# A new instruction order at the head of an MLP, and a last output tile stored in two halves

## The reference

```python
def _moe2_ref(x, w_in, w_out) -> np.ndarray:      # x 2304x512, w_in 512x2048, w_out 2048x512
    h = x @ w_in
    g = np.maximum(0.01 * h, h)
    return (g @ w_out).astype(np.float32)
```

## Time and profile before

| | us |
|---|---|
| median of 3 runs (lowest, highest) | 390.22 (389.74, 390.31) |
| the profiled execution | 390.76 |
| its span, first to last instruction | 389.0 |
| TensorE busy in the span | 376.5 |
| DVE busy | 220.4 |
| ACT busy | 195.0 |

### The profile page before, as it was taken

The page is one execution under the profiler, slowest core; times in us unless marked ns, Lnnn a source line. Parts: engine busy times, 40 slices in busy tenths (PEclk is TensorE's granted clock), DMA queues, the critical chain, the costliest instruction groups (busy, mean ns, idle before and its releaser), DMA issues.

```text
span 389.0 us, 9358 instructions
## 1 busy us (share of the span) xinstructions
PE 376.5 (97%) x3515; PEld 288.0 (74%) x3515; DVE 220.4 (57%) x763; ACT 195.0 (50%) x527; POOL 12.5 (3%) x46
## 2 busy tenths in 40 slices
PE   5999999999999999789999999999999999999996
PEld 3788877867785333467888888888888888888885
DVE  6776576665574273397866444644464464445443
ACT  5888878778762012476644334334334434433431
POOL 1200000000000100021100000000000000000000
PEclk9999999999999999999999999999999999999999
DMA  7798789769999999980000100200020002002002
GB/s 250 274 335 303 258 277 318 260 243 348 396 383 386 386 386 386 385 304 4 3 0 35 48 0 1 83 0 0 2 82 0 3 0 81 2 0 82 2 1 81
DMA packets 27214, 62.09 MB, mean 160 GB/s; under 512 B 2081, under 2 KB 2593, under 8 KB 27169
## 3 DMA queue, kind: packets, MB, share of 16 engines
q1 hardware_dynamic: 27024, 61.33, 43.8%
q10 hardware_dynamic: 144, 0.16, 0.1%
HBM read 56.77 MB, written 4.72 MB: 158 GB/s over the span
## 4 chain that ended last, share of the span: by engine, by line
PE 89%; DMA 5%; DVE 3%; SPq 1%; ACT 1%; issue 1%; POOL 0%; DVEq 0%; ACTq 0%; POOLq 0%
PE bank L862 10%; PE bank L864 10%; PE bank L863 10%; PE turned L557 6%; PE bank L590 6%; PE bank L533 6%; PE turned L863 6%; PE turned L864 6%; PE turned L862 5%; PE bank L579 5%; PE bank L847 4%; PE bank L763 4%; DMA slot<-in_moe_w_out_dram 3%; PE turned L607 3%; PE bank L873 1%; DMA qk<-in_k_dram 1%
## 5 line engine op out<-in xcount | busy, mean ns | idle before, releaser
L1457 DVE SCALAR_TENSOR_TENSOR g_sb<-bank,h_sb 128x384 f32<-128x384 f32 x93 | 51.8, 557 | 93.6 <-ACT h_sb L1133 93.4
L1133 ACT COPY h_sb<-bank 128x384 f32<-128x384 f32 x93 | 44.5, 478 | 118.9 <-PE bank L847 118.6
L864 PE MATMUL bank<-w_hi,g_lo 128*128 128x512 f32 x180 | 70.9, 394 | 0.0
L862 PE MATMUL bank<-w_hi,g_hi 128*128 128x512 f32 x180 | 70.6, 392 | 0.1
L863 PE MATMUL bank<-w_lo,g_hi 128*128 128x512 f32 x180 | 70.7, 393 | 0.0
L959 ACT ACTIVATE prob<-prob,row_min 128x192 f32<-128x192 f32 (+1 forms) x144 | 51.9, 440 | 3.9 <-DVE row_min L1211 3.9
L1464 DVE TENSOR_TENSOR g_lo<-g_sb,g_hi 128x384 fp32r<-128x384 f32 x93 | 51.0, 549 | 0.1
L1138 ACT CAST g_hi<-g_sb 128x384 fp32r<-128x384 f32 x93 | 48.0, 516 | 0.2 <-DVE g_sb L1457 0.2
L967 ACT COPY probT<-turned 128x384 f32<-128x384 f32 (+1 forms) x76 | 33.4, 443 | 20.2 <-PE turned L557 19.1
L533 PE MATMUL bank<-qk 64*64 64x192 f32 (+2 forms) x576 | 35.8, 325 | 5.1 <-DMA qk<-in_q_dram 4.0
L862 PEld LDWEIGHTS bank<-w_hi,g_hi 128*128 128x128 f32 x180 | 33.8, 188 | 9.1 <-DVE g_lo L1464 1.7
(11 more groups left out here) (169 smaller groups left out, 435.2 us busy)
## 6 DMA issues: line engine op xcount, KB each, us to landing
slot<-in_moe_w_dram SPq DMA_DIRECT2D x22, 1024.0 KB, 8.5
slot<-in_moe_w_dram SPq DMA_DIRECT2D x5, 2048.0 KB, 16.0
v<-in_v_dram SPq DMA_DIRECT2D x16, 325.0 KB, 4.5
qk<-in_q_dram SPq DMA_DIRECT2D x15, 288.0 KB, 4.6
qk<-in_k_dram SPq DMA_DIRECT2D x15, 288.0 KB, 5.3
slot<-in_moe_w_in_dram SPq DMA_DIRECT2D x4, 1024.0 KB, 14.3
slot<-in_moe_w_out_dram SPq DMA_DIRECT2D x8, 512.0 KB, 11.7
out_dram<-o_sb SPq DMA_DIRECT2D x5, 768.0 KB, 3.6
```

The lines of the kernel that those rows point to most:

```text
L862: nc.tensor.matmul(acc, hi, w_hi[:, f, :], start=(f == 0), stop=False)
L864: last = nc.tensor.matmul(acc, lo, w_hi[:, f, :], start=False, stop=(f == FT - 1))
L1133: nc.scalar.copy(h_sb[:, f % 2, :], bank[6 + f % 2][:, 0:GW]).then_inc(h_copied, 1)
L1457: nc.vector.scalar_tensor_tensor(out=g_sb[:, f % 2, :], in0=bank[6 + f % 2][:, 0:GW], scalar=0.01, in1=h_sb[:, f % 2, :], op0=ALU.mult, op ...
```

## The change

At the head of the MLP: TensorE runs `project(0)` ahead of `combine_T(3)`, no longer behind it. On ACT both halves of the first w_out pair are rounded later: half 0 behind g pieces 0 and 1, half 1 behind the h copy of block 1; g pieces 2, 3 and 4 are taken one place earlier each or more. On DVE the residual of half 0 moves behind the leaky of block 0 and g piece 2; pieces 3 and 4 move ahead of the leaky of blocks 1 and 2.

At the end: the last two blocks of the last group run tile by tile (tile 0 gets its 6 matmuls, then tile 1, then tile 2), DVE copies the last tile in two halves of 256 columns, SP stores the first half and ACT the second.

```diff
@@ sync, the last group's stores
-                sp.dma_start(out[row0:row0 + P, :], o_sb[:, t, :]).then_inc(out_stored, 16)
-            sp.wait_ge(out_stored, 16 * (NG - 1 + GT))
+                cols = slice(0, DM // 2 if t == GT - 1 else DM)
+                sp.dma_start(out[row0:row0 + P, cols], o_sb[:, t, cols]).then_inc(out_stored, 16)
+            sp.wait_ge(out_stored, 16 * (NG + GT))
@@ tensor
-            pe.wait_ge(c_hi_done, 3)
-            pe.wait_ge(c_lo_done, 3)
-            combine_T(3, C_BANK[3])
             project(0)
+            pe.wait_ge(c_hi_done, 3)
+            pe.wait_ge(c_lo_done, 3)
+            combine_T(3, C_BANK[3])
             project(1)
+            def last_blocks(par):
+                for t in range(GT):
+                    for f in (FT - 2, FT - 1):
+                        if t == 0:
+                            pe.wait_ge(glo_done, (NG - 1) * FT + f + 1)
+                        for kind in range(3):
+                            g, w = ((g_hi, w_hi), (g_hi, w_lo), (g_lo, w_hi))[kind]
+                            last = nc.tensor.matmul(bank[GT * par + t][:, :], g[:, f % NR2, t * P:(t + 1) * P], w[:, f, :],
+                                                    start=False, stop=(f == FT - 1 and kind == 2))
+                    last.then_inc(acc_done, 1)
-                        down(grp, par, FT - 2)
-                        down(grp, par, FT - 1)
+                        last_blocks(par)
@@ scalar
-            split_w_first(0)
                 split_g(0)
                 split_g(1)
-                split_w_first(1)
+                split_w_first(0)
+                split_g(2)
+                split_g(3)
                 act.wait_ge(h_done, 1)
...
-                split_g(2)
+                split_g(4)
                 copy_h(1)
-                split_g(3)
+                split_w_first(1)
                 round_g(1)
                 copy_h(2)
                 split_w(1)
                 round_g(2)
-                split_g(4)
                 split_g(5)
...
+            act.wait_ge(acc_copied, GT * NG + 1)
+            act.dma_start(out[NG * GW - P:NG * GW, DM // 2:DM], o_sb[:, GT - 1, DM // 2:DM]).then_inc(out_stored, 16)
@@ vector
-                    nc.vector.tensor_copy(o_sb[:, t, :], bank[GT * par + t][:, :]).then_inc(acc_copied, 1)
+                    parts = 2 if known(grp) and grp == NG - 1 and t == GT - 1 else 1
+                    for i in range(parts):
+                        cols = slice(i * DM // parts, (i + 1) * DM // parts)
+                        nc.vector.tensor_copy(o_sb[:, t, cols], bank[GT * par + t][:, cols]).then_inc(acc_copied, 1)
                 split_g(0)
                 split_g(1)
-                split_w_first(0)
...
                 split_g(2)
+                split_w_first(0)
                 lower_g(0)
+                split_g(3)
                 leaky(1)
                 split_w_first(1)
-                split_g(3)
                 lower_g(1)
+                split_g(4)
                 leaky(2)
                 split_w(1)
                 lower_g(2)
-                split_g(4)
                 split_g(5)
```

## The result

Over 20 executions each the median is 389.08 us for the changed kernel and 391.5 for the one before; the ratio is 0.9934 with a 95% interval of 0.9917 to 0.9952, so 0.66% faster (0.48 to 0.83%). The forecast was 388.07 of 390.22, a ratio of 0.9945, inside that interval. In microseconds the two lie 1.0 apart: the forecast started from the median of three executions, 390.22, and over 20 that kernel's median is 391.5. The gain is 2.4 us by these medians, 2.15 was forecast. The profiled execution took 388.57 with a span of 386.8, where 388.6 and 386.85 were forecast from the profile before.

What follows compares the result with a forecast made beforehand. TensorE was taken as the bound, except in the MLP's first blocks, where other engines' order makes it wait, and after its last matmul. Head 2.0 plus tail 0.15 us made 2.15, from 390.22 to 388.1 us; range 387.4 to 389.3.

Steps and rivals of the forecast that it cites:

- steps 1 to 3: MLP head: earlier `project(0)` and ACT g pieces bring `up(0)` 0.55 us and the first product 0.75 us earlier.
- the loads don't pin the gain: MLP head: w_out part 2 lands near 167.0, ACT reaches it at 169.9, so loads don't limit the 2.0 us.
- step 3: First block: no weight residual ahead of the leaky, so the first product comes at 164.26 instead of 165.01.
- steps 4 and 5: First blocks: second product group stalls 0.22 us; g piece 3 ahead of `leaky(1)` brings `up(3)` 2.02 us earlier.
- POOL's doubling: MLP head: POOL's doubling of g piece 3 ends by 166.9, letting `up(3)` go at 166.93.
- step 7: Blocks 4 and 5: late DVE residuals stall TensorE 0.22 and 0.37 us; block 5 keeps 2.03 us of gain.
- Tail: Kernel end: split copies lose 0.1 to 0.17 us, the half-size last store gains 0.34; net 0.15 us taken.
- the wait for block 15's residual: Last blocks: wait moves behind three matmuls, with 0.1 us cover; if that is gone, it costs under 0.1 us.
- DVE as the bound: MLP head: later DVE instructions give back half, leaving a head gain of 1.0 us, time 389.1; chance 0.2.
- The split tail: Kernel end: two copies and a second queue's landing come 0.3 to 0.6 us later, time 388.6; chance 0.1.
- the slow small store: Kernel end: last small store takes 5.4 us to landing instead of 2.1, time 391.7; chance 0.03.
- the gain tied to a fixed time: First group: a load or late stall takes back the whole head gain, time 390.2 or little below; chance 0.05.

Runs made afterwards that it cites:

- pieces-back run: Changed kernel with DVE's g pieces 3 and 4 again behind the weight residuals of blocks 1 and 2; ratio to the kernel before 0.9971.
- filled kernel: Kernel before with 12 identity transposes put into TensorE's waits for `up(0)` and the first product; 391.49 us, ratio to before 1.0002.
- combine back: Changed kernel with `combine_T(3)` ahead of `project(0)` again; 389.66 us, ratio to the kernel before 0.996.
- head alone: New order at the head with the old end of the kernel before; 390.01 us, ratio to before 0.996.
- residual early: Changed kernel with DVE's residual of w_out half 0 ahead of the first leaky; ratio to the kernel before 0.9945.
- residual and `up(1)` early: Changed kernel with DVE's residual of w_out half 0 ahead of the first leaky and `up(1)` ahead of the first products; 389.14 us, ratio to before 0.9953.

## Why the prediction was right, step by step

**Projection, pieces, first product (steps 1 to 3)** came as laid out: `project(0)` at 160.11 (160.2), ACT's pieces at 161.25 (161.35), `up(0)` at 162.72 (162.7), first product at 164.26 (164.26). The gain at the first product is 0.68 from the anchor, where I had 0.75, and it holds for this pair of traces; about 0.3 of it hangs on when the load of w_out lands, since the old head has its first product at 5.53 and 5.54 in the traces where the load came earlier. I had written that the loads don't pin the gain. They don't hold up the new order, but the old one waits for one of them, so they set a part of what the change is worth. Where the load is early, the place of `combine_T(3)` is the whole gain at the first product: 5.57 with it back, 5.53 with the whole old head. The residual moved behind the first leaky, to which step 3 points, brings nothing there: moved back ahead of it, in the new order, the first product stays at 5.16.

**`up(3)` (steps 4 and 5)**, 166.95 against 166.93, is the largest step, as I said, and the pieces-back run shows it alone: 1.39 us with two DVE instructions. I had 1.1 there. I had POOL's doubling end near 166.9; it ended at 166.54, and the time came out all the same because TensorE was busy with its third group until then.

**What DVE gives back (step 7)** was mis-sized: I had stalls of 0.22 and 0.37 before blocks 4 and 5. There is none before block 4 and next to none before block 5 (they start at 175.43 and 177.69, not 175.32 and 177.94). 0.33 of the 0.59 is that TensorE itself was later at `up(6)`, 175.25 and not 174.92: groups of three behind a wait or a projection took 0.93 to 0.96, where I had laid out the steady rate. The other 0.26 is DVE, whose residual of block 5 ended at 177.63 and not 177.89:

```profile
177.08 0.55 DVE L1480 TENSOR_TENSOR g_lo<-g_sb,g_hi 128x384 fp32r<-128x384 f32 x1
```

So block 5 was 2.28 earlier, not 2.03; 0.07 of that is the earlier anchor, which leaves 2.21. `up(15)` keeps 2.06: most of the rest went inside block 5, whose second matmul came 0.34 behind its first instead of 0.22. The stall late in the group is in both traces.

**That the sum met the span to 0.05 us is luck in part.** The head was 2.06 and the tail 0.25, both above what I took, and the earlier anchor gave 0.07 more; against that, the matmuls between `up(15)` and the last one took 0.18 longer (last section), for which my sum had nothing. 2.06 + 0.25 + 0.07 - 0.18 is the 2.2 by which the span is shorter.

**Tail.** 0.25 us of the 0.15 taken. The split copies cost 0.06 (0.76 for both; they ended 1.18 us behind the last matmul's start, against 1.12), where I had 0.1 to 0.17, and the landing was 0.3 shorter (1.8 for 2.1), as taken. The turns of the tiles cost nothing and bring at most 0.06; the wait for block 15's residual did not stall. The second queue brings about 0.1, which my sum didn't have as a term of its own: it is the 0.04 by which SP issues later and the 0.07 by which its issue is longer. By the rule of the Trainium skill that I quoted (DMA: Bandwidth & Descriptors, "Issuing engines are not separate DMA queues") a second issuing engine saves the sequencer's time to issue and no more; the traces agree, as the landing takes 1.80 us behind SP's last issue and 1.82 behind ACT's.

**The rivals.** DVE as the bound, with half of the head's gain given back, did not come: the head brought 1.7 to 2.1 us, not 1.0. There is something in it, as DVE is busy 8.15 of 9.20 us there, and moving 0.69 us of its work into a wait brought 0.2. The split tail gained 0.25 instead of losing 0.3 to 0.6, and the slow small store and the gain tied to a fixed time did not occur.

**What the sum lacked** is the clock, which I had only looked up in the one trace before, where it was full. Its fall is seen in 34 of 80 executions of the old head. I can't say how much of the measured 0.66% it is: the filled kernel, without falls, is no faster than the one before. Taking only executions at the full clock, the medians are 390.9 us before (46, from the three later rounds) and 389.1 changed (28), 1.8 us or 0.45%; this is no paired comparison.

## What to carry to other kernels

Where several engines feed the first blocks of a pipeline, write down for each instruction on the busiest helper engine who waits for it next, and run the short ones with a waiting reader ahead of the long ones without: two moved pieces of 0.3 us were worth 1.4. A wait for a load belongs behind whatever is ready without it; here that was worth 0.1 us at the first product when the load was early, and about 0.3 more when it was late. At the very end, halve the last copy and store; it is worth a quarter of a microsecond, and a gain that small is to be read from fixed points of a trace, as executions spread by far more.

## What the runs showed of the hardware

**The clock falls behind short waits, and in some executions only.** The same program has a mean granted clock of 0.998 to 1.00 in some executions and 0.994 to 0.996 in others, 34 of 80; in the three traces that have it, it falls behind the waits between `project(1)` and the first product (0.38 and 1.3 us). The trace before had waits of 0.68 and 1.31 us there and kept the full clock. Twelve small transposes in these waits took it to 0 of 12, though the 1.1 us wait at `up(3)` stayed. One wait of 1.10 alone, in the changed kernel, gave 4 of 32; with the 0.38 ahead of it (combine back) it is 9 of 13. In the three other timed kernels with that one wait (head alone, pieces back, residual early) it is 1 of 36. What else decides in which execution it falls was not tried.

**The same matmuls at the same granted clock take different time.** From `up(15)` to the last matmul all kernels run the same number of matmuls, with no idle to speak of. It took 186.00 us in one trace (residual and `up(1)` early), 186.09 before, 186.27 in the changed kernel and 186.57 with the head alone, which is why the last matmul moved by 1.88 from the anchor where `up(15)` moved by 2.06. The spread is 0.6 us in traces whose clock reads 1.000, more than twice the tail's gain. It builds up in small steps: of the 80 times from one `up` to the next in the five later groups, 75 are 2.24 us in the trace before (the other 5 are 2.40), and with the head alone only 36 are, while 39 are 2.25 or 2.26. The cause stays open.
